# Rounding weights on ScalarE instead of GpSimd in the first batch, and subtracting in pieces

## The reference

```
scores = cap * tanh(q @ k.T / sqrt(64) / cap)
attn = exp(scores - max) / (sum + 1e-9)
x = attn @ v, heads side by side               # 1792 x 768
x = (sigmoid(x @ w_gate) * (x @ w_val)) @ w_out  # 768 -> 1536 -> 768
h = x @ w_in                                   # 768 -> 2048
y = (h * cos(h)) @ w_out2                      # 2048 -> 768
```

## Time and profile before

| | before |
|---|---|
| median of 3 runs | 1307.53 us (1307.04 to 1308.49) |
| the profiled execution | 1308.7 us, span of the trace 1306.9 us |
| mean granted TensorE clock | 0.991 |
| TensorE busy | 1266.8 us (97%) |
| VectorE, ScalarE, GpSimd busy | 716.9, 569.1, 400.4 us (55%, 44%, 31%) |
| batch 0's attention alone | 0 to about 107 us |
| batch 0: product 1, 2, 3, 4 | from about 107, 201, 285 and 345 us |
| batch 1 starts | 442 us |

### The profile page before, as it was taken

One profiled execution on the slowest core, in us unless ns is written; L12 is line 12 of the kernel. 1 busy time (PEld: TensorE's weight loads), 2 busy tenths in 40 slices (PEclk: granted clock), 3 DMA queues, 4 the chain that ended last, 5 costly groups with the idle time before them and its releaser, 6 DMA issues.

```text
span 1306.9 us, 17361 instructions
## 1 busy us (share of the span) xinstructions
PE 1266.8 (97%) x6468; PEld 1138.3 (87%) x6468; DVE 716.9 (55%) x1249; ACT 569.1 (44%) x1085; POOL 400.4 (31%) x394
## 2 busy tenths in 40 slices
PE   7899998999899999999999999999999999999999
PEld 5557997889888999999999999999999999999998
DVE  6993438868887312786676511487667621113620
ACT  5881135545654212665665311566565411103610
POOL 4526887758976001340042000341022100000000
PEclk8999999999999999999999999999999999999999
DMA  3327896658865567654675366754685456666673
GB/s 96 82 80 262 326 326 239 204 193 303 321 245 222 199 217 246 201 166 166 231 253 194 132 224 227 239 176 147 218 283 179 151 196 217 217 218 217 228 243 127
DMA packets 115812, 274.84 MB, mean 210 GB/s; under 512 B 32784, under 2 KB 35856, under 8 KB 115728
## 3 DMA queue, kind: packets, MB, share of 16 engines
q1 hardware_dynamic: 112128, 268.22, 59.6%
q10 hardware_dynamic: 3600, 5.51, 1.1%
HBM read 214.70 MB, written 58.98 MB: 209 GB/s over the span
## 4 chain that ended last, share of the span: by engine, by line
PE 84%; DVE 9%; ACT 4%; issue 2%; DMA 0%; POOL 0%; POOLq 0%; ACTq 0%
PE acc L421 23%; PE acc L422 23%; PE acc L423 23%; PE t_ps L360 5%; DVE prob L714 3%; PE s_ps L351 3%; PE s_ps L352 3%; PE acc L369 2%; PE acc L370 2%; ACT prob L554 2%; PE acc L383 1%; DVE tmp_b L810 1%; DVE rowmax L702 1%; DVE tmp_b L807 1%; DVE h_lo L819 1%
## 5 line engine op out<-in xcount | busy, mean ns | idle before, releaser
L421 PE MATMUL acc<-h_hi,w_hi 128*128 128x448 f32 x672 | 256.9, 382 | 0.0
L422 PE MATMUL acc<-h_lo,w_hi 128*128 128x448 f32 x672 | 246.8, 367 | 0.0
L423 PE MATMUL acc<-h_hi,w_lo 128*128 128x448 f32 x672 | 246.6, 367 | 0.0
L421 PE MATMUL acc<-x_hi,w_hi 128*128 128x448 f32 x576 | 210.7, 366 | 0.0
L422 PE MATMUL acc<-x_lo,w_hi 128*128 128x448 f32 x576 | 210.4, 365 | 0.0
L423 PE MATMUL acc<-x_hi,w_lo 128*128 128x448 f32 x576 | 210.4, 365 | 0.0
L785 DVE TENSOR_TENSOR tmp_b<-acc,tmp_a 128x448 f32<-128x448 f32 x48 | 30.0, 624 | 229.8 <-PE acc L423 229.6
L554 ACT ACTIVATE prob<-prob,shift,cap_abs 112x448 f32<-112x448 f32 x192 | 144.1, 752 | 5.1 <-DVE shift L704 4.5
L421 PE MATMUL acc<-z_hi,w_hi 128*128 128x448 f32 x384 | 140.3, 365 | 1.0 <-DVE z_lo L797 1.0
L423 PE MATMUL acc<-z_hi,w_lo 128*128 128x448 f32 x384 | 140.2, 365 | 0.0
L422 PE MATMUL acc<-z_lo,w_hi 128*128 128x448 f32 x384 | 140.2, 365 | 0.0
(11 more groups left out here) (77 smaller groups left out, 2018.3 us busy)
## 6 DMA issues: line engine op xcount, KB each, us to landing
w_hi<-w_pair SPq DMA_DIRECT2D x156, 384.0 KB, 3.0
w_lo<-w_pair SPq DMA_DIRECT2D x156, 384.0 KB, 3.8
qk_raw<-qk SPq DMA_DIRECT2D x48, 448.0 KB, 4.9
w_raw<-w SPq DMA_DIRECT2D x52, 384.0 KB, 4.7
w_pair<-w_hi SPq DMA_DIRECT2D x52, 384.0 KB, 2.3
w_pair<-w_lo SPq DMA_DIRECT2D x52, 384.0 KB, 3.3
w_hi<-w_pair SPq DMA_DIRECT2D x36, 512.0 KB, 3.3
w_lo<-w_pair SPq DMA_DIRECT2D x36, 512.0 KB, 4.5
```

What stands on the lines that cost most here:

```text
L421: e.matmul(out[:, 0:S], w_hi[p][:, wb, :], a_hi[:, kb, :], start=first, stop=False)
L422: e.matmul(out[:, 0:S], w_hi[p][:, wb, :], a_lo[:, kb, :], start=False, stop=False)
L423: return e.matmul(out[:, 0:S], w_lo[p][:, wb, :], a_hi[:, kb, :], start=False, stop=last)
```

## The change

In batch 0 ScalarE rounds the weights of units 2 to 17 (products 1 and 2) and 26 to 31 (product 4), both halves of unit u while it works on unit u - 1. In product 1 this stands at the head of its unit, in products 2 and 4 between the second tanh and exp 0, and for unit 26 at the head of the last unit of product 3. GpSimd waits for it on a new semaphore (`s_wact`) and only subtracts, in pieces of two blocks (256 columns). Units 0 and 1 and product 3's stay as they were. In product 4 the store of the unit before now comes behind the rounding in ScalarE's queue.

```diff
+    def high_by_scalar(u):
+        return 2 <= u < OFF3 or u >= OFF4
+    def highs_before(u):
+        return u - 2 - (U3 if u >= OFF4 else 0)
...
                         for h in range(2):
-                            part = slice(h * HALF_MAX, h * HALF_MAX + blk)
+                            at = h * HALF_MAX
                             e.wait_ge(s_wld[p][h], 16 * (uses + 1))
-                            rounded(w_hi[p][:, part, :], w_raw[p][h][:, 0:blk, :]).then_inc(s_whi, 1)
-                            e.wait_ge(s_whi, 2 * u + h + 1)
-                            rest(w_lo[p][:, part, :], w_raw[p][h][:, 0:blk, :], w_hi[p][:, part, :]).then_inc(s_wsplit, 1)
+                            if high_by_scalar(u):
+                                e.wait_ge(s_wact, 2 * highs_before(u) + h + 1)
+                                for k in range(0, blk, 2):
+                                    m = rest(w_lo[p][:, at + k:at + k + 2, :], w_raw[p][h][:, k:k + 2, :], w_hi[p][:, at + k:at + k + 2, :])
+                                m.then_inc(s_wsplit, 1)
+                            else:
+                                rounded(w_hi[p][:, at:at + blk, :], w_raw[p][h][:, 0:blk, :]).then_inc(s_whi, 1)
+                                e.wait_ge(s_whi, 2 * (u if u < 2 else u - OFF3 + 2) + h + 1)
+                                rest(w_lo[p][:, at:at + blk, :], w_raw[p][h][:, 0:blk, :], w_hi[p][:, at:at + blk, :]).then_inc(s_wsplit, 1)
...
+            def weight_high(u):
+                if not high_by_scalar(u):
+                    return
+                p, blk = u % 2, blocks_of[stage_of(u)]
+                e.wait_ge(s_acc, 2 * (u - 1) + 2 * CREDIT)
+                e.wait_ge(s_wkept[p], 64 * (u // 2))
+                for h in range(2):
+                    part = slice(h * HALF_MAX, h * HALF_MAX + blk)
+                    e.wait_ge(s_wld[p][h], 16 * (u // 2 + 1))
+                    e.activation(w_hi[p][:, part, :], w_raw[p][h][:, 0:blk, :], ACT.Copy).then_inc(s_wact, 1)
...
+                def next_high(j):
+                    if is_first(b) and off + j + 1 < UNITS:
+                        weight_high(off + j + 1)
...
                 def unit1(j, p, i, peeled):
+                    next_high(j)
...
-                        beside_parts(i, *beside_unit(2, b, j, p, i, peeled))
+                        beside_parts(i, *beside_unit(2, b, j, p, i, peeled), after_tanh=lambda: next_high(j))
...
                 def unit3(j, p, i, peeled):
                     m = b * KF2 + 2 * j
+                    next_high(j)
...
+                    def after_tanh():
+                        next_high(j)
+                        if j > 0:
+                            store(j - 1, 1 - p)
+
+                    beside_parts(U2 // 2 + i, *beside_unit(4, b, j, p, i, peeled), after_tanh=after_tanh)
```

More of the change, by code:

```diff
@@ L107, in build @@
     s_whi, s_wsplit, s_held = sem("w_hi_done"), sem("w_split"), sem("gpsimd_waits_held")
+    s_wact = sem("w_hi_done_by_scalar")
     s_wpair = [[sem(f"w_pair_loaded{p}{h}") for h in range(2)] for p in range(2)]
@@ L142, in is_first, with stage_of @@
         return b == 0
+    def high_by_scalar(u):
+        return 2 <= u < OFF3 or u >= OFF4
+    def highs_before(u):
+        return u - 2 - (U3 if u >= OFF4 else 0)
+    def stage_of(u):
+        return next(s for s in (1, 2, 3, 4) if u < units_of[s][1] + units_of[s][0])
     def pair_uses(stage, b, i):
@@ L241, in keep @@
             def keep(u):
-                stage = next(s for s in (1, 2, 3, 4) if u < units_of[s][1] + units_of[s][0])
+                stage = stage_of(u)
                 j, blk, p = u - units_of[stage][1], blocks_of[stage], u % 2
@@ L653, in unit4 @@
                         return
-                    first = isinstance(j, int) and j == 0
-                    beside_parts(U2 // 2 + i, *beside_unit(4, b, j, p, i, peeled),
-                                 after_tanh=None if first else lambda: store(j - 1, 1 - p))
+                    def after_tanh():
[3 more added lines that the diff above has]
+                    beside_parts(U2 // 2 + i, *beside_unit(4, b, j, p, i, peeled), after_tanh=after_tanh)
                     if isinstance(j, int) and j == U4 - 1:
```

## The result

| | kernel before | changed kernel |
|---|---|---|
| median of 6 runs | 1306.35 us (1305.38 to 1308.49) | 1315.97 us (1311.85 to 1320.2) |
| ratio | | 1.0071, 95% interval 1.0047 to 1.0096 |
| profiled execution, span | 1308.7, 1306.9 us | 1312.65, 1310.9 us |
| mean granted clock, profiled | 0.991 | 0.992 |
| ScalarE, GpSimd, VectorE busy | 569.1, 400.4, 716.9 us | 601.5, 373.7, 688.9 us |

The change makes the kernel slower. It does what it says: GpSimd is busy 27 us less and VectorE 28 us less, ScalarE 32 us more. Measured twice more among the experiments, it was 0.43% (0.30 to 0.57%) and 0.47% (0.31 to 0.63%) slower than the kernel before, which is 6.1 and 7.3 us. Those two have more runs of the kernel before beside them (17 and 26 instead of 6), so 6 to 7 us is the better figure for the loss, and the first 9.6 us is its upper end.

A forecast was written before the change was run, and what follows sets the result against it. TensorE bounds the kernel (84% of the chain), with some 20 us of its idles in play. Waits +8.1 less passages 1.4 and 1.2 gave +5.5 us: 1314.2 profiled, 1313 against the median; range 1304 to 1321.

The forecast's parts named there:

- ScalarE's rounding ahead of exp 0: Products 2 and 4, ScalarE's queue: two half roundings put 1.5 and 1.9 us ahead of exp 0.
- The lock: VectorE's chain to `pt_lo` of block 2: three locking instructions wait for GpSimd's pieces, 0.78 to 1.49 us extra, 1.13 taken.
- The ten waits: TensorE before L369, five units each of products 2 and 4: 2.48 and 1.65 us lost per unit, 20.7 us; net +8.1.
- The passages: Product 2's start and product 4's first unit: TensorE's idles there shrink, gaining 1.4 and 1.2 us.
- The clock: Half clock behind TensorE's idles in batch 0: four more such stretches, +2 us (0 to 6), left out of the forecast.
- Half clock after most of the new idles: Rival, TensorE's idles in batch 0: eight of twelve bring half clock instead of three, 1323 us; chance 0.13.
- The even exchange: Rival, VectorE's chain: longer ScalarE queue and shorter locks cancel, extra 0.4 to 0.8 us, 1308.5 us; chance 0.18.
- the gain by the lock alone: Rival, VectorE's chain: VectorE hardly waits in a row of pieces, so the kernel gets faster, 1299.5 us; chance 0.14.
- The cover of batch 1's first weights: End of batch 0: 2 to 6 of the 13 us until batch 1's first weights are used are taken, costing nothing.

The follow-up runs named there:

- e1_late: Changed kernel with ScalarE's rounding in products 2 and 4 moved behind exp 3 instead of ahead of exp 0; 1294.15 us, ratio 0.9881 to the kernel before.
- e6_mid: Changed kernel with ScalarE's rounding in products 2 and 4 moved to between exp 1 and `pt_hi` of block 2; 1295.82 us, ratio 0.9903 to the kernel before.
- e8_blocks: Changed kernel with GpSimd's subtractions in pieces of 128 columns instead of 256; 1307.44 us, ratio 0.9993 to the kernel before.

## Why the prediction was right

The direction was right, and the forecast of 1313 is 3 us below the median of 1316 and 1 and 3 us below the two later ones (1313.9 and 1316.4). As a difference the forecast was +5.5 us, and +9.6, +6.1 and +7.3 were measured. The mechanism was right too; that the sum came so close is in part luck, as the steps show:

- **ScalarE's rounding ahead of exp 0.** 1.5 and 1.9 us were forecast; exp 0 started 1.47 us late in product 2 and 1.89 in product 4 (two roundings from 359.63, exp 0 at 361.52). The middle of the two slopes gave 0.82 and 1.02 us a half and the rows have 0.832 and 1.048. The rule of the Trainium skill ("ScalarE: Activation LUTs", What ACT_TABLE_LOAD costs), 186 ns and 0.833 a column, makes an estimated 0.826 and 1.039: the trace agrees, and it was the tighter figure. That this place in the queue is the cause is shown by e1_late and e6_mid: the same work a little later, and 17 to 18 us of waits are gone.
- **The lock.** An extra of 1.13 us was assumed in VectorE's chain. From exp 0 at 220.41 to TensorE's start at 225.12 are 4.71 us; less the 3.37 of batch 1 and 0.04 that is an extra of 1.30 us, the same in all five units of product 2, and 1.10 in those of product 4 (4.51 us). e8_blocks cuts 1.30 to 0.55 with pieces of half the width. The Trainium skill ("SBUF — State Buffer", Who interferes with whom) says of who locks: copies, casts and scalar forms can take both ports, reductions never do, and whoever issues first holds them for the whole instruction. The trace agrees: the guard took 0.77 us instead of 0.17 against a piece, and VectorE's row maximum 1.07 to 1.09 us in all 96 of its instructions. Between two back-to-back instructions of GpSimd the rows have VectorE getting in each time, and that is what the pieces live on. GpSimd lost little by it: its six pieces ran 4.34 us, 0.72 us each, with three of VectorE's locking instructions among them; 0.71 each was forecast.
- **The ten waits.** Forecast 5 x 2.48 + 5 x 1.65 = 20.7 us with the 0.16 us that a record hides; in the same count they measure 20.6 + 10 x 0.16 = 22.2. Product 2 was within 0.15 us a unit. In product 4 the first unit was mis-sized: TensorE reached its L387 3.6 us after the second tanh, not 4.8 as in the fifth unit, so it waited 2.67 us. The order written out for that unit has five blocks of the product between the scores and this point, where the others have seven, and two blocks are 1.2 us. In the kernel before this did not show: TensorE ran at half clock there and came to its L369 5.4 us behind exp 0 (358.69 to 364.10). Net +9.6 us instead of +8.1.
- **The passages.** Product 2's start gained 2.4 us (0.79 left of 3.23), where 1.4 were forecast: VectorE's last pair of scalings took 1.17 us instead of 1.43 and ended at 198.8, not 199.5. In product 4 the tanh's 3.75 us went and the forecast wait at the first weights came, 2.21 us at 351.49: 1.5 gained, 1.2 forecast. Sum of the idles: 9.6 - 2.4 - 1.5 = +5.7 us, against a forecast of +5.5. Here is the luck: the waits were 1.5 us too low and the gains 1.3 us too low, and the two errors cancel.
- **The clock** was priced at +2 us (0 to 6), by four half-clock stretches more than before, and left out of the forecast. In the 5 us right behind its idles the one trace of the kernel before shows three such stretches (0.66, 0.66 and 0.50, 5.9 us of work) and three traces of the changed kernel show two, four and four (3.4, 6.8 and 6.8 us): -2.5 to +0.9 us net. The new waits bring half clock, and the two idles that are gone took theirs away, which the price of +2 did not count. By these few traces leaving the term out was right. With it the +4.0 us of the profiled execution are accounted for: 5.7 - 2.5, and 0.7 of difference in the stretches where both kernels do the same work.
- **Rivals.** Half clock after most of the new idles did not come: four of twelve at most, where eight were needed. The even exchange and the gain by the lock alone did not come either, both for the reason given: GpSimd's next piece is ready each time, and the extra was 1.1 to 1.3 us, not 0.4 to 0.8 or nothing. The cover of batch 1's first weights held; batch 1 started at 445.9 in the profiled execution instead of 442.2, and these 3.7 us are the idles less the clock.

Left open: why the clock falls behind one idle of 2.45 us and not behind the next, and why the first measurement gave 9.6 us and not the 6 to 7 of the later ones. Its six runs of the changed kernel went from 1311.85 us at a clock of 0.992 to 1320.2 at 0.988, and only the fastest but one has a trace.

## What to carry to other kernels

When work is moved to an idle engine, the busy share says little; what counts is the place in that engine's queue and what stands behind it. Here 1.5 us of ScalarE's work ahead of exp 0 cost 2.5 us a unit of product 2, and two exps later 0.2 to 0.5. And look at each half of a change alone: the pieces on GpSimd were worth 1.3% by themselves, and the move to ScalarE, in the place where it stood, took that and more away. And a cost of the clock is read on both sides of a comparison: the new idles brought half clock, and the old ones that vanished had brought as much.

## What the runs showed of the hardware

- Two GpSimd instructions back to back left VectorE a turn between them, even with no gap: in product 2 the guard took 0.76 to 0.78 us against pieces of 0.74 us, so it waited for the rest of one piece and not for the row of six. With three blocked VectorE instructions in a row, pieces 0.28 us shorter made the chain 0.75 us shorter.
- A scalar operation on 112x2 elements is blocked like one on 112x448 (0.77 us instead of 0.17); the reciprocal beside it is not (0.17 us in all 96).
- Idles of TensorE cost more than their length when half clock follows. In three traces of the changed kernel it followed 10 of 21 idles of 1.90 to 2.67 us and none of 12 idles of 1.44 to 1.48 us. Filling the idles with matmuls of no use made this kernel 6.0 us faster at a mean clock of 0.995 instead of 0.991.
